# Reordering the first pass of a fused kernel: merges before the next set's grams, masks before inverse steps

## The reference, cut to what matters

```python
# 1: a delta rule over 768 steps, for 4 x 8 heads of width 48
k_n = k / (norm(k) + 1e-6)
for t in range(768):
    y[t] = q[t] @ state
    state = state + beta[t] * outer(k_n[t], v[t] - k_n[t] @ state)
# 2: feed-forward layer on x = y as 3072 rows of 384
h = x @ w_in                    # 384 x 2048
x2 = maximum(0.01 * h, h) @ w_out
# 3: one expert of 8 for each row
logits = x2 @ w_gate + modality_bias[modality_id]
e = argmax(logits); p = softmax(logits)[e]
out = p * (maximum(x2 @ w1[e], 0) @ w2[e])
```

## Time and profile before

| | |
|---|---|
| median of 3 runs | 948.14 us (947.1 to 948.7) |
| profiled execution | 945.98 us, span 944.2 us |
| mean granted clock of TensorE | 0.943 of full speed |
| first matmul of `up(0, 0)` | 101.25 us |
| first matmul of set 1's merges | 144.84 us |

### The profile page before, as it was taken

One profiled execution on the slowest core, in us unless ns is written; L12 is line 12 of the kernel. 1 busy time (PEld: TensorE's weight loads), 2 busy tenths in 40 slices (PEclk: granted clock), 3 DMA queues, 4 the chain that ended last, 5 costly groups with the idle time before them and its releaser, 6 DMA issues.

```text
span 944.2 us, 26960 instructions
## 1 busy us (share of the span) xinstructions
PE 841.5 (89%) x10528; PEld 744.1 (79%) x10529; DVE 569.7 (60%) x1598; ACT 352.2 (37%) x613; POOL 87.1 (9%) x100
## 2 busy tenths in 40 slices
PE   2665399999999999999999999999879999999962
PEld 2555388888888888888888887888768989898852
DVE  5937897888777877787779633445623333333350
ACT  4562236443543454445443523225112222222230
POOL 1000000000010001000000010010311121212220
PEclk8865699999999999999999999999989999999985
DMA  8931354237415641664155133171241111111121
GB/s 127 319 70 22 70 139 96 69 76 140 68 46 107 122 70 31 119 125 70 30 105 110 34 70 77 43 210 43 65 155 42 34 50 34 45 38 34 43 83 68
DMA packets 148308, 77.92 MB, mean 83 GB/s; under 512 B 112496, under 2 KB 144240, under 8 KB 147824
## 3 DMA queue, kind: packets, MB, share of 16 engines
q1 hardware_dynamic: 143264, 66.59, 32.4%
q0 software_dynamic: 4096, 9.48, 3.3%
q10 hardware_dynamic: 848, 0.39, 0.2%
HBM read 59.30 MB, written 13.21 MB: 77 GB/s over the span
## 4 chain that ended last, share of the span: by engine, by line
PE 76%; DMA 5%; DVE 5%; ACT 5%; SPq 3%; issue 3%; ACTq 1%; DVEq 0%; POOL 0%; POOLq 0%
PE bank L551 19%; PE bank L532 17%; PE bank L643 11%; PE bank L618 10%; PE bank L628 2%; PE bank L481 2%; PE bank L453 2%; PE bank L443 2%; PE bank L513 1%; PE bank L464 1%; PE bank L517 1%; ACT gram_d L1038 1%; PE bank L433 1%; DMA wo_lo<-wo_lo_d 1%; SPq L807 1%
## 5 line engine op out<-in xcount | busy, mean ns | idle before, releaser
L551 PE MATMUL bank<-wo_hi,g_hi 128*128 128x392 f32 x384 | 136.1, 354 | 3.3 <-DVE g_lo L1484 1.9
L551 PE MATMUL bank<-wo_lo,g_hi 128*128 128x392 f32 x384 | 130.9, 341 | 0.0
L551 PE MATMUL bank<-wo_hi,g_lo 128*128 128x392 f32 x384 | 130.8, 341 | 0.0
L532 PE MATMUL bank<-x_hi,wi_hi 128*128 128x512 f32 x288 | 119.2, 414 | 13.0 <-DVE x_lo L1475 12.3
L1111 ACT ACTIVATE g_raw<-bank 128x512 f32<-128x512 f32 x96 | 57.4, 597 | 158.5 <-PE bank L532 158.3
L1479 DVE SCALAR_TENSOR_TENSOR g_raw<-g_raw 128x512 f32<-128x512 f32 x96 | 66.0, 688 | 83.6 <-ACT g_raw L1111 80.2
L532 PE MATMUL bank<-x_hi,wi_lo 128*128 128x512 f32 x288 | 114.0, 396 | 0.0
L532 PE MATMUL bank<-x_lo,wi_hi 128*128 128x512 f32 x288 | 113.9, 395 | 0.0
L1118 ACT ACTIVATE g_hi<-g_raw 128x512 fp32r<-128x512 f32 x96 | 60.7, 633 | 97.0 <-DVE g_raw L1479 97.0
L1484 DVE TENSOR_TENSOR g_lo<-g_raw,g_hi 128x512 fp32r<-128x512 f32 x96 | 66.0, 688 | 31.2 <-ACT g_hi L1118 30.0
L643 PE MATMUL bank<-w_hi,ht_hi 128*128 128x384 f32 x200 | 72.5, 363 | 8.4 <-DVE ht_lo L1788 6.4
(11 more groups left out here) (215 smaller groups left out, 1455.2 us busy)
## 6 DMA issues: line engine op xcount, KB each, us to landing
wo_lo<-wo_lo_d SPq DMA_DIRECT2D x80, 196.0 KB, 2.6
w_raw<-in_moe_w SPq DMA_DIRECT2D x6, 1536.0 KB, 8.5
x_rows<-stage SPq DMA_DIRECT2D x6, 770.0 KB
kq_in_rows<-in_k SPq DMA_DIRECT2D x6, 768.0 KB, 7.0
k_raw<-in_k SPq DMA_DIRECT2D x24, 192.0 KB
vals<-in_v SPq DMA_DIRECT2D x48, 96.0 KB, 2.8
kq_in_rows<-in_q SPq DMA_DIRECT2D x6, 768.0 KB, 6.9
x_raw<-y_t SPq DMA_DIRECT2D x33, 96.0 KB, 2.4
```

The costliest lines, as they stand in the source:

```text
L532: mm = pe.matmul(bank[0][:], a[:, m, P * f:P * f + P], x[:, m, :], start=(m == 0 and x is x_hi and a is wi_hi), stop=(m == KT - 1 and a is ...
L551: mm = pe.matmul(acc[i][:, 0:DX], g[f % 2][:, P * i:P * i + P], w, start=(f == 0 and k == 0), stop=(f == FT - 1 and k == 2))
```

## The change

- TensorE, slots n = -1: the merges follow the gate weights directly. `gram_k(1, 0)` stands behind `merge_p`, `gram_k(1, 1)` ahead of `old_values`, `gram_q(0, 1)` behind `old_values`, and the outputs of both chunks behind the second `updates`.
- The QK steps of set 0 get fixed banks (2 to 4 and 0) and leave the turn; the last two KK steps swap banks. `gram_q(0, 0)` waits for `wx_rdy`, since bank 2 held the gate weights, and `up(0, 0)` for the last mask of set 0.
- ScalarE: the halves of `w_in` and the grams of set 1 are spread anew, three halves behind `begin_x`; `roots(1)` goes from slot 12 to slot 10, ahead of `copy_y(0, 1)`.
- VectorE: `rest_gate_weights` goes to slot 5, the masks of chunk 1 to slot 8, the last gram of set 1 to slot 9, `norm(1)`, `scale_gram(1)` and inverse steps 0 to 4 to slot 10. Slots 12 to 15 hold nine steps instead of eighteen and slots (0, 0) to (0, 3) seventeen instead of thirteen.
- `token_biases` is VectorE's first work of the slots; SyncE issues its loads right behind the first keys.

```diff
-INV_FIRST = {-2: {13: (0, 12), 14: (12, 24), 15: (24, INV)}, -1: {12: (0, 5), 13: (5, 10), 14: (10, 14), 15: (14, 18)}}
+INV_FIRST = {-2: {13: (0, 12), 14: (12, 24), 15: (24, INV)}, -1: {10: (0, 5), 12: (5, 8), 13: (8, 10), 14: (10, 12), 15: (12, 14)},
+             0: {0: (14, 18), 1: (18, 22), 2: (22, 26), 3: (26, INV)}}
...
-PLACED = {("KK", 0, 1, 0): 5, ("KK", 0, 1, 1): 6, ("KK", 1, 0, 0): 5, ("KK", 1, 0, 1): 6, ("KK", 1, 1, 0): 3, ("KK", 1, 1, 1): 7}
+PLACED = {("KK", 0, 1, 0): 5, ("KK", 0, 1, 1): 6, ("KK", 1, 0, 0): 5, ("KK", 1, 0, 1): 6, ("KK", 1, 1, 0): 7, ("KK", 1, 1, 1): 3,
+          ("QK", 0, 0, 0): 4, ("QK", 0, 0, 1): 5, ("QK", 0, 1, 0): 6, ("QK", 0, 1, 1): 7}
...
@@ TensorE, gram_q @@
+                if (t, c) == (0, 0):
+                    pe.wait_ge(s.wx_rdy, 1)
@@ TensorE, slot @@
-                    pe.wait_ge(*is_drained(("KK", 1, 1, 1)))
+                    pe.wait_ge(*is_drained(("QK", 0, 1, 1)))
                     up(0, 0)
...
                         merge_p(n + 1, 1)
+                        if n < 0:
+                            gram_k(1, 0)
...
                     if f == 8:
+                        if n < 0:
+                            gram_k(1, 1)
                         old_values(n + 1, 1)
+                        if n < 0:
+                            gram_q(0, 1)
+                    if f == 9:
+                        updates(n + 1, 1)
                         if n < 0:
                             outputs(0, 0, 0)
                             outputs(0, 0, 1)
-                    if f == 9:
-                        updates(n + 1, 1)
-                        if n < 0:
-                            gram_q(0, 1)
                             outputs(0, 1, 0)
                             outputs(0, 1, 1)
...
                     gate_weights()
-                    gram_k(1, 0)
-                    gram_k(1, 1)
@@ SyncE: the loads of beta, keys and values go behind those of w_gate, bias and mod_raw @@
@@ ScalarE, slot @@
                         copy_diag(n + 1)
+                        if n < 0:
+                            split_wi(0)
...
                         copy_p(n + 1, 1)
+                        if n < 0:
+                            copy_gram(1, 0, 0)
...
                         if n < 0:
+                            split_wi(1)
+                            split_wi(2)
                             copy_gram(1, 1, 0)
-                            for p in range(1, 4):
-                                split_wi(p)
...
+                    if f == 10:
+                        copy_y(n + 1, 0, 0)
+                        copy_y(n + 1, 0, 1)
                         if n < 0:
-                            for p in range(4, 2 * KT):
-                                split_wi(p)
+                            roots(1)
...
                             begin_x()
+                            for p in range(3, 2 * KT):
+                                split_wi(p)
@@ VectorE, slot @@
-                half = 0 if n == -1 and f == 12 else min(1, len(inv))
+                half = 0 if n == -1 and f in (10, 12) else min(1, len(inv))
...
+                    if f == 5 and n < 0:
+                        rest_gate_weights()
...
-                    if f == 9 and n < 0:
+                    if f == 8 and n < 0:
                         mask_q(0, 1, 0)
                         mask_q(0, 1, 1)
...
+                if n == -1 and f == 9:
+                    copy_gram(1, 1, 1)
+                    split_wi(1)
+                    split_wi(2)
+                    turn_gram(1)
                 if n == -1 and f == 10:
-                    copy_gram(1, 1, 1)
-                    turn_gram(1)
+                    norm(1)
+                    scale_gram(1)
                 if n == -1 and f == 11:
-                    rest_gate_weights()
-                    token_biases()
+                    for p in range(3, 2 * KT):
+                        split_wi(p)
...
+            token_biases()
             for n, f in slots():
                 slot(n, f)
```

More of the change, by code:

```diff
@@ L52 @@
           0: (18, 21), 1: (21, 25), 2: (25, 29), 3: (29, INV)}
-INV_FIRST = {-2: {13: (0, 12), 14: (12, 24), 15: (24, INV)}, -1: {12: (0, 5), 13: (5, 10), 14: (10, 14), 15: (14, 18)}}
+INV_FIRST = {-2: {13: (0, 12), 14: (12, 24), 15: (24, INV)}, -1: {10: (0, 5), 12: (5, 8), 13: (8, 10), 14: (10, 12), 15: (12, 14)},
+             0: {0: (14, 18), 1: (18, 22), 2: (22, 26), 3: (26, INV)}}
 def steps_at(n, f):
     if f >= 10:
-        return n + 2, range(*INV_FIRST.get(n, INV_AT).get(f, (0, 0)))
-    return n + 1, range(*INV_AT.get(f, (0, 0))) if n >= 0 else range(0)
+        return n + 2, range(*(INV_FIRST[n] if n < 0 else INV_AT).get(f, (0, 0)))
+    return n + 1, range(*(INV_FIRST[0] if n == 0 else INV_AT).get(f, (0, 0))) if n >= 0 else range(0)
 class Region:
@@ L880, in _ @@
             load_rows(k, 0)
[L881 to L885, removed]
             sp.wait_ge(s.wg_zero, 1)
@@ L892, in _ @@
                              ).then_inc(s.misc_in, 16)
+            for hh in range(2):
+                for odd in range(2):
+                    sp.dma_start(beta_rows[odd::2, :, hh ^ odd, :], beta_d[odd, hh]).then_inc(s.beta_in, 16)
+            load_keys(0)
+            load_values(0)
             for n, f in slots():
@@ L1183, in slot @@
                         if n < 0:
+                            split_wi(1)
+                            split_wi(2)
                             copy_gram(1, 1, 0)
-                            for p in range(1, 4):
-                                split_wi(p)
-                    if f == (8 if n < 0 else 10):
-                        copy_y(n + 1, 0, 0)
-                        copy_y(n + 1, 0, 1)
                     if f == 9:
@@ L1230, in slot @@
                             copy_gram(n + 2, 1, 0)
-                    if f == (9 if n >= 0 else 12):
+                    if f == (9 if n >= 0 else 12) and n != -1:
                         roots(n + 2)
@@ L1241, in slot @@
                     gate_weights()
-                    copy_gram(1, 0, 0)
-                    split_wi(0)
                 if n >= -1 and 0 <= j + 2 < FT:
@@ L1724, in slot @@
                 if n == -1 and f == 12:
-                    norm(1)
                     split_x(0)
@@ L1729, in slot @@
                     add_s(n + 1, 1, 1)
-                if n == -1 and f == 12:
-                    scale_gram(1)
                 for i in inv[half:]:
@@ L1735, in slot @@
                     inverse_out(n + 1)
-                if n == -1 and f in (7, 8, 9, 10):
-                    for p in {7: (0,), 8: (1, 2), 9: (3, 4), 10: (5,)}[f]:
-                        split_wi(p)
+                if n == -1 and f == 7:
+                    split_wi(0)
                 if n >= -1 and 0 <= j + 2 < FT:
```

## The result

The changed kernel takes 937.61 us (median of 4 runs, 933.5 to 939.88), the one before 947.62 (4 runs, 947.04 to 948.7): a ratio of 0.9888, interval 0.9852 to 0.9924, 10.0 us less. The forecast was 936.5, within 932.5 to 941.0. The profiled execution took 933.5 us, 12.5 less than that of before, against 11.6 forecast; it is the fastest of its four.

The account below looks back on a forecast made before the run. TensorE's waits bound the first stretch, VectorE the second, up to 144.84 us. Gains of 8.6 + 3.0 = 11.6 us took the profiled 945.98 to 934.4; the median, 2.2 above, was forecast at 936.5, range 932.5 to 941.0.

Parts of the forecast that it names:

- The clean border: At 144.84 us, where TensorE becomes busy 151.90 of 155.16 us: work brought forward there brings the end forward equally.
- First stretch: TensorE from 47 to 101 us, pass over set 0: up(0, 0) starts at 92.65 instead of 101.25, 8.6 us gained.
- Steps 2 to 6: Set 0, from the pause through merge_p, gram_q and old_values to the outputs of both chunks, ending at 79.85 us.
- Step 8: From copy_y's end at 81.2 to x_hi, 7.78 us as before, so up(0, 0) starts at 92.65.
- The pause: TensorE's unexplained 3.33 us wait, read as late instructions behind weight loads; now inside merge_p, the rest starting at 52.72.
- The rival without a pause: merge_p starts at 49.8 and ends at 53.4, all behind it 2.8 us sooner; 933.7 us, chance 0.20.
- Second stretch: From up(0, 0) to merge_x of set 1, decided by VectorE's path: 3.0 us gained, mask wait 5.99 to about 2.4.
- Without idle from about 99.5: Sign of being right: VectorE has no idle time from about 99.5 to 132.7 us.
- the stretch gives nothing: Rival for up(0, 0) to set 1's merges: VectorE loses its saving or TensorE stalls; 939.5 us, chance 0.18.
- nothing either way: VectorE's token biases leave a wait for x and go into 8.38 us of idle before 13.56: no gain or loss.
- the slower rival: Late token-bias loads delay VectorE, costing from a landing at 14.7 us on; 951.8 us at 30, chance 0.06.
- one sign of being wrong: VectorE's first copy of the gram coming later than 13.6 us.

Follow-up runs that it names:

- biases back: Changed kernel with token_biases back in VectorE's slot (-1, 11) and their loads back behind beta, keys and values: 940.8 us, ratio 0.9909.
- quiet merges: Changed kernel with all feed-forward weight loads, the list and the queries of set 1 issued only behind merge_p: 961.65 us (1 run).
- steps into gaps: Changed kernel with two more inverse steps in slot (-1, 12) and slot (-1, 13)'s two between leaky and rest_g: 937.1 us, ratio 0.9853.
- masks ahead of inverse steps, alone: Kernel before with only the masks of set 1 moved ahead of inverse steps, later steps in slots (0, 0) to (0, 3): 966.97 us, ratio 1.0002.
- groups 1 and 3: Follow-up runs on two other chips, each including the unedited changed kernel: 954.32 and 954.29 us; kernel before 966.43 and 965.57.
- group 2: Follow-up runs on one further chip, including the unedited changed kernel: 941.87 us; kernel before 951.75.

## Why the prediction was right

- **The clean border.** From 144.84 us on nothing else had to move, and the rest is 799.4 and 799.5 us.
- **First stretch, 8.6 us forecast, 9.8 measured.** The start of the merges was 0.9 us later than forecast (47.98). "The load of the queries still leaves at 19.78" was wrong: it left at 20.45, the queries were used from 27.39 instead of 26.60, the next keys' load left at 31.09 instead of 30.30, and the delay stayed. Part of it is the new order of the first loads, as *biases back* shows (first keys 0.2 to 0.5 us later in every execution); how much of the 0.9 can't be told, since it also varies between executions of one kernel. Steps 2 to 6 then held within 0.8 us at every landmark: main merge_p 53.44 (52.72), gram_q 61.33 (60.65), old_values 67.48 (66.75), the second outputs 76.04 (76.15), end of copy_y 81.02 (81.2). Where the start was 0.9 late and the end 0.2 early, TensorE's clock gave part of it: it was granted 0.98 from 66.5 to 69.9 us, and old_values took 1.15 us instead of 1.96. The forecast had the lower clock throughout, so this part was luck.
- **Step 8 mis-sized.** The 7.78 us from copy_y to x_hi were taken over as they stood; they measured 6.68. They are ScalarE's issue (4.72 us in the profile before, 3.70 here) and some 3 us behind it, for the transfer or the splits. The term that varies is the issue. The change did nothing to shorten it; that this execution drew a short one is luck too, 1.0 us of it.
- **The pause** was read rightly as bound to a place in the stream and to the loads, as *quiet merges* shows; "at the same place of the stream and time" was nearly so. Over the changed kernel's executions it ended at 53.44 to 56.06 us, but always behind 135 matmuls (133 in the old order), and 5.5 to 6.1 us after the start of merge_x: the place is in the stream, not at a fixed time of the execution. The rival without a pause is refuted.
- **Second stretch, 3.0 forecast, 2.8 measured.** The mask wait came at 2.49 (2.4 forecast), the merges at 132.22 (132.9). The counts behind the 2.4 were off: behind the first `rest_g` the first mask came after 4 steps and the second after 6, not 6 and 8 (before, 9 and 13). TensorE was ready at 131.2 (131.0 forecast). Its clock rose 16 us after `up(0, 0)`, sooner than before (19 us), so the loss of 0.3 us that was set aside for it did not come. "Without idle from about 99.5" held, but most of 2.8 us of idle around its start (1.33 and 1.48) had been left unused; *steps into gaps* made 2.0 us of them. That the stretch gives nothing is refuted; the 5.99 us wait was never worth its length, since VectorE was busy 41.32 of 43.59 us, and a mask moved ahead pushes the steps behind it nearer to the merges, as *masks ahead of inverse steps, alone* shows.
- **Token biases, "nothing either way": wrong in its reason.** In the new order VectorE has as much work as ScalarE ahead of x. Where they used to stand they cost up to 1.4 us when the issue is short. Their loads were in at 9.45 us, so the slower rival never came near. But one sign of being wrong did show: VectorE's first copy of the gram came at 13.98, later than 13.6. It waited for TensorE, whose first keys were late behind the moved loads, and not for the biases.
- **The median** gained 10.0 us where the profiled execution gained 12.5: 933.5 was the fastest of four that spread over 6.4 us, before's over 1.7. The issue accounts for up to 2 us of such a spread; what makes the rest was not traced and stays open. That the forecast of 936.5 missed the median by only 1.1 us is in part luck: the profiled execution was 0.9 better than forecast, and the median lay 4.1 above it instead of the 2.2 assumed.

## What to carry to other kernels

A block of many small instructions that runs beside large loads stopped here for 2 to 4 us at a fixed place of the stream. Moving work did not take the stop away, but one can choose what is behind it: put the block ahead whose results other engines can work on meanwhile. A long wait for a late piece is not its price: look who is busy throughout the stretch, and fill that engine's idle pieces. And a transfer's path begins at its issue: here five small transfers from one queue cost 3.7 to 5.8 us, more than the 3 us of their landing.

## What the hardware showed unexpectedly

On the chips of groups 1 and 3 the same kernels take 12 to 19 us longer than in group 2 and in the first measurement, nearly all behind the merges of set 1 (the rest column). In the passes that follow, TensorE stops in `outputs` for no reason that an engine gives. The waits of TensorE from 140 to 620 us, in the changed kernel in group 3 and then in the first measurement (total, times, longest):

```profile
PE bank L517 <- issue: 5.0, 10, 1.2
PE bank L521 <- issue: 2.5, 6, 0.5
```

```profile
PE bank L517 <- issue: 1.5, 1, 1.5
```

That is 7.5 us against 1.5, mostly in pieces of 0.4 to 0.5, and so 6 of the 18 us by which the rest differs. With the stops come drops of the granted clock to a mean of 0.91 over 360 to 380 and 460 to 480 us, where the first measurement has 1.00. The old order has the stops too (7.1 us with the masks alone moved, in group 1), so they go with the chip and not with the change. They look like the pause above, but no run shows what fetches late there, and none shows where the other 12 us are.
